# Narrower stationary operands in the capacity search, two more of its steps ahead of the expert stream, and a new table of spacings

## What is computed

```
def _moe2_ref(x, w_gate, w1, w2) -> np.ndarray:
    N, D = x.shape
    E = w_gate.shape[1]
    cap = N // E
    logits = x @ w_gate
    flat = logits.flatten()
    order = np.argsort(-flat)
    assigned = -np.ones(N, dtype=np.int64)
    counts = np.zeros(E, dtype=np.int64)
    for idx in order:
        tok, e = (int(idx) // E, int(idx) % E)
        if assigned[tok] >= 0 or counts[e] >= cap:
            continue
        assigned[tok] = e
        counts[e] += 1
        ...
    out = np.zeros((N, D), dtype=np.float32)
    for e in range(E):
        mask = assigned == e
        h = np.maximum(x[mask] @ w1[e], 0.0)
        out[mask] = h @ w2[e]
    return out.astype(np.float32)
```

## Time and profile before

| | us |
|---|---|
| median of 3 runs | 829.41 |
| lowest and highest | 829.33, 831.57 |
| profiled execution, its own time | 829.41 |
| its span, first to last instruction | 825.4 |
| PE busy | 727.5 |
| DVE busy | 359.0 |

### The profile page before, as it was taken

How to read it: one execution, slowest core, us unless ns; L and a number is a source line. 1 busy time by engine, 2 the same in 40 slices (tenths; PEclk the granted TensorE clock), 3 DMA queues, 4 the chain that set the end, 5 groups by cost and what they waited for, 6 DMA issues and landing times.

```text
span 825.4 us, 13873 instructions
## 1 busy us (share of the span) xinstructions
PE 727.5 (88%) x4561; PEld 504.0 (61%) x4561; DVE 359.0 (43%) x1458; ACT 220.7 (27%) x685; POOL 192.3 (23%) x251
## 2 busy tenths in 40 slices
PE   3788998998299999997219999999999999999995
PEld 2788988998287678675115555455555545555552
DVE  3577786886411121122583726537273563600000
ACT  2677787884011111111001111110211111021210
POOL 8275645452111111111010020202102020211001
PEclk9799999999599999999557999999999999999998
DMA  9898987587691618800033521507043160642000
GB/s 212 188 207 201 224 205 173 134 213 238 223 382 35 232 32 322 315 8 3 6 126 119 191 90 50 220 13 255 25 166 109 33 243 14 254 174 105 30 0 38
DMA packets 130466, 119.88 MB, mean 145 GB/s; under 512 B 95858, under 2 KB 95858, under 8 KB 130224
## 3 DMA queue, kind: packets, MB, share of 16 engines
q1 hardware_dynamic: 118192, 88.45, 35.2%
q10 hardware_dynamic: 6464, 14.73, 5.9%
q0 software_dynamic: 5760, 16.03, 5.7%
HBM read 105.95 MB, written 16.50 MB: 148 GB/s over the span
## 4 chain that ended last, share of the span: by engine, by line
PE 78%; DVE 9%; issue 3%; SPq 3%; DMA 3%; POOL 1%; ACT 1%; ACTq 0%; POOLq 0%; DVEq 0%
PE bank L1121 21%; PE bank L1136 21%; PE bank L1017 9%; PE bank L1034 8%; PE bank L877 3%; PE bank L898 3%; PE bank L1062 2%; PE bank L920 2%; SPq L465 2%; PE bank L887 2%; PE bank L1094 1%; DVE scratch L1346 1%; DVE shared L1357 1%; PE bank L997 1%; PE bank L864 1%
## 5 line engine op out<-in xcount | busy, mean ns | idle before, releaser
L1121 PE MATMUL bank<-scratch,weights 128*128 128x384 f32 x512 | 177.4, 499 | 0.7 <-ACT scratch L1302 0.7
L1136 PE MATMUL bank<-weights,scratch 128*128 128x512 f32 x384 | 175.2, 600 | 0.0
L1121 PEld LDWEIGHTS bank<-scratch,weights 128*128 128x128 f32 x512 | 94.3, 192 | 64.3 <-issue 9.8
L1136 PEld LDWEIGHTS bank<-weights,scratch 128*128 128x128 f32 x384 | 69.6, 190 | 70.7 <-issue 68.4
L1205 ACT ACTIVATE scratch<-shared,neg_max 128x120 f32<-128x120 f32 x192 | 73.4, 383 | 33.0 <-DVE neg_max L1357 20.9
L1308 ACT ACTIVATE scratch<-bank 128x384 f32<-128x384 f32 x64 | 31.4, 491 | 152.8 <-PE bank L1121 152.8
L664 POOL TENSOR_TENSOR scratch<-scratch,row_inv 128x480 f32<-128x480 f32 x48 | 47.3, 986 | 78.7 <-DVE row_inv L1367 78.5
L1017 PEld LDWEIGHTS bank<-mix,weights 128*128 128x128 f32 x512 | 60.8, 197 | 5.2 <-issue 5.2
L1017 PE MATMUL bank<-mix,weights 128*128 128x128 f32 x512 | 61.7, 279 | 1.5 <-DVE mix L1571 1.5
L822 POOL DMA_INDIRECT out<-scratch,idx x24 | 25.2, 1049 | 147.4 <-ACT scratch L1314 145.6
L1034 PE MATMUL bank<-weights,mix 128*128 128x512 f32 x128 | 58.2, 597 | 0.0
(11 more groups left out here) (225 smaller groups left out, 941.6 us busy)
## 6 DMA issues: line engine op xcount, KB each, us to landing
weights<-in_moe_w SPq DMA_DIRECT2D x20, 2048.0 KB, 8.3
scratch<-in_moe_w SPq DMA_DIRECT2D x8, 2048.0 KB, 15.5
weights<-in_moe_w ACTq DMA_DIRECT2D x16, 512.0 KB, 6.1
mix<-in_v SPq DMA_DIRECT2D x40, 192.0 KB
rows<-row SPq DMA_DIRECT2D x24, 264.5 KB, 3.6
weights<-in_k SPq DMA_DIRECT2D x24, 256.0 KB, 5.2
scratch<-in_q SPq DMA_DIRECT2D x24, 256.0 KB, 4.4
weights<-in_v ACTq DMA_DIRECT2D x24, 192.0 KB, 4.1
```

What stands on the lines that cost most here:

```text
L1121: last = mm(hb2[f % 2][:, 0:CAP], w1_sb[odd][:, c, f * P:(f + 1) * P], xT2[odd][:, c, :], start=(c == 0), stop=(c == C - 1), skip_group_ch ...
L1136: last = mm(yb2[c % 2][:, :], hT2[odd][:, f, c * P:(c + 1) * P], w2_sb[odd][:, f, :], start=(f == 0), stop=(f == FC - 1), skip_group_check ...
```

## The change

Four edits, all in the second mixture.

```
@@ -349,7 +349,7 @@
-        reach = row_hot
+        reach = row_hot[:, :, 0:KEYS, :]
@@ -1059,7 +1059,7 @@
-                        last = mm(counts[:, 0:E], reach[:, j // 2, :, j % 2], cand_h[:, j, :],
+                        last = mm(counts[0:ROUND_KEYS[r], 0:E], reach[:, j // 2, 0:ROUND_KEYS[r], j % 2], cand_h[:, j, :],
                                   start=(j == 0), stop=(j == NT - 1), skip_group_check=True)
@@ -1095,10 +1095,10 @@
-            AHEAD = 4
+            AHEAD = 6
             UP, DOWN = 3, 4
             TURN_AT = CT * FC - 6
-            spacing = [20, 9, 10, 6] + [14, 6] * (ROUNDS - 2) + [12, 12, 13, 17]
+            spacing = [18, 7, 8, 7] + [12, 8] * (ROUNDS - 2) + [15, 11, 8, 17]
@@ -1592,7 +1592,6 @@
             v_.memset(room_e, float(CAP))
-            v_.memset(reach, 0.0)
             link(v_.memset(assigned, 0.0))
@@ -1680,12 +1679,11 @@
                         plink(ins)
+                        v_.tensor_copy(digits_h[:, 0, :], digits_i[:, 0, :])
+                        plink(v_.tensor_scalar(digits_h[:, 1:, :], digits_i[:, 1:, :], 1.0, None, ALU.add))
                     dve.wait_ge(s.counted, 2 * ROUNDS * ph + 2 * r + 1)
                     v_.tensor_tensor(out=enough_h[0:wide_r, :], in0=counts[0:wide_r, 0:E], in1=room_e[0:wide_r, :],
                                      op=ALU.is_ge).then_inc(s.judged, 1)
-                    if r == 0:
-                        v_.tensor_copy(digits_h[:, 0, :], digits_i[:, 0, :])
-                        plink(v_.tensor_scalar(digits_h[:, 1:, :], digits_i[:, 1:, :], 1.0, None, ALU.add))
```

## The result

The changed kernel takes 864.84 us (median of 4 runs, 862.97 to 865.60) against 830.28 us for the kernel before in the same comparison. The ratio is 1.041, with a 95% interval of 1.039 to 1.043: 34.6 us slower, where 26.0 us had been forecast, and above the range, which ended at 862.

A forecast was written before the change was run, and what follows sets the result against it. TensorE's instructions bound the stream, and TensorE and VectorE taking turns bound the prelude. Terms 4.2 + 0.5 + 4.5 - 0.6 + 10.2 + 7.2 = +26.0 us on 829.41 gave 855.4 us, range 838 to 862.

The forecast's parts named there:

- Edit 1: Narrower count loads cost more on TensorE: +10.2 us in the stream, +4.2 us in the prelude before the added round.
- the fast load is lost: Count matmuls: bf16 loads of fewer than 128 columns lose the fast path; slow load with clock as it is, chance 0.62.
- Edit 2: No zeroing: the 1.34 us VectorE memset is covered by the transfer of the scores, so 0.
- Edit 3: Conversions earlier, ahead of round 0's judgement: about +0.25 us in phases 0 and 1, +0.5 us together; stream 0.
- Edit 4: AHEAD = 6: a whole round ahead of expert 0's transposes adds 4.5 us; its count and vote leave the stream, -0.6 us.
- Worth 1 us either way: Low-clock stretch of the first products: a shift in where the clock rises changes the time by 1 us.
- Edit 5: New spacings stall the stream 0.35 and 0.65 us before steps 11 and 12 in six phases, plus 1.2: +7.2 us.
- The vote of round 0: In the stream, a down product (0.88 us) between count and vote hides the judgement's wait behind the conversions: 0.
- the load keeps its price: Rival: narrow count loads cost no more than 128-column ones, +10.5 us, 840 us; chance 0.17.
- The clock did not rise in the prelude: Judges the rival that slow prelude counts lift the clock from 0.50 to 1.00: -8, 847 us; chance 0.09.
- overlapping loads: Rival: narrow count loads run beside the matmul ahead; at 5 ns per matmul in the stream, 827 us; chance 0.02.

The follow-up runs named there:

- e2: Kernel before with only the narrower count operand and no zeroing: 852.74 us against 829.65, ratio 1.027.
- e1: Changed kernel with count matmuls back at 128 stationary columns and the zeroing back: 840.28 us against 829.65 for the kernel before.
- e7: Kernel before with counts of 32, 64, 128, 128 and 128 stationary columns, zeroing kept: 840.13 us against 836.13, ratio 1.005.
- e5: Kernel before with only the two conversions of round 0 moved ahead of the wait for the counts: 836.37 us against 836.13.
- e12: Second run of the kernel before with only the round-0 conversions moved earlier: 833.35 us against 833.22, ratio 1.001.
- e9: Kernel before, unchanged, run again on the second chip: 832.74 us against 833.22, ratio 1.000.
- e4: Kernel before with only AHEAD raised from 4 to 6, old spacings, full width: 830.66 us against 829.65, ratio 1.003.
- e3: Kernel before with only the new table of spacings, AHEAD = 4: 833.55 us against 829.65, ratio 1.006.
- e11: Kernel before with the new spacings and AHEAD = 6 together, full width, late conversions: 841.51 us against 833.22, ratio 1.010.
- e10: Changed kernel, no further edit, run again on the second chip: 865.63 us against 833.22 for the kernel before, ratio 1.038.
- e13: Kernel before with the vote of round 0 one down product later (spacing 13, not 9): 833.27 us against 836.25, ratio 0.996.

## Why the prediction was wrong

The direction was right, and so were the mechanisms in the sum, but the price of the narrow loads was too low and some costs were missing from it; the total was 8.6 us short of the measured 34.6, or 6.4 short of the 32.4 on one chip, and the range missed by 3 us. Term by term, from the traces of the changed kernel:

- **Edit 1, "half the f32 price: 50 ns at full clock, 100 ns at half clock, for 127 columns; half of that for 63 (25 and 50); no change for 31."** This step failed in its size. Measured: (1.56 - 0.20) / 23 = 59 ns and (2.72 - 0.24) / 23 = 108 ns for 127 columns, (0.96 - 0.17) / 23 = 34 ns and (1.44 - 0.19) / 23 = 54 ns for 63. At full clock a group of 24 gains 0.81 us, not 0.60, and 63 and 31 columns gain 0.30 and 0.09 us, not 0. In the stream that is 17 x 0.81 + 5 x 0.30 + 5 x 0.09 = 15.7 us for the 10.2 forecast, the largest part of the miss; in the prelude 3 x 1.38 + 2 x 0.5 = 5.1 for 4.2. The products beside the 31- and 63-column counts add the 1.1 us of e2, for 0 forecast. I had halved a price that was itself read off rows with 17 and 120 moving columns, and had put 56 ns no further out than the edge. At full clock the pace goes from 34 ns for 63 columns to 59 for 127, so 64 columns make 25 ns; 127 at that rate are 49 ns, close to the 50 forecast, and some 10 ns do not go by the width. At half clock it goes from 54 to 108 ns, with next to nothing over. What the 10 ns are, no run here shows.
- **That the fast load is lost** was right, and e1, e2 and e7 show it. By the rule of the Trainium skill (TensorE: Matmul & The Clock Gate, section Weight-path perf modes — Fast Weight Load (FWL) and DoubleRow) only 128 weights of a type other than FP32 load fast; the rows of 31, 32, 63, 64, 127 and 128 columns agree in that only 128 keeps the old price of a count. The gain that the section gives, about twofold, is 59 against 25 ns here at full clock; at half clock the trace has more, 108 against 26.
- **Edit 2, 0** and **Edit 3, +0.5.** The zeroing was covered, VectorE now waits 7.20 us for the scores in place of 5.32. The conversions cost 0.3 us in each of phases 0 and 1, as forecast (e1 has both without a late signal); the late signal adds 0.5 us in phase 1. In their times e5 and e12 can't be told from before.
- **Edit 4, +4.5 in the prelude, -0.6 in the stream.** The transposes come 5.10 us after the vote of round 1 (451.83 - 446.73) where it was 0.35 before, so +4.75 (against e9, whose transposes waited 0.53 us for their rows, +4.4). "Worth 1 us either way" for the clock was too narrow: e4 gained 2.6 us by it.
- **Edit 5, stalls of 0.35 and 0.65 us.** From step 10 to 11 the trace has 475.99 - 473.61 = 2.38 us where three products take 2.03, and from 11 to 12 it has 2.66: 0.35 and 0.63. In expert 5 the stall ahead of step 12 of phase 7 is 0.73 us of idle time, 0.8 us from start to start, and not 1.2; the six phases and this one lose 6.7 us for the 7.2 forecast. The place and size held; that the table works only together with AHEAD was in the positions, but unsaid, and e3 and e11 show it.
- **The vote of round 0** was not in the sum. "TensorE has a down product (0.88 us) between count and vote there: 0" fails with 0.5 us of idle time in five phases, 3.1 us from start to start. It is no cost of the change where before has it as well, but counts against the changed kernel where the comparison is with a run that has it not.

Together, from the first count to the end:

- The first pair of traces, prelude: 5.1 for the counts, 0.6 for the conversions, 0.5 for the late signal, 4.75 for the added round, and 0.5 between step 11 of phase 0 and the first count of phase 1, which e2 has too, which no term foresaw and whose cause is open. In all 11.45 us, measured 11.4.
- The first pair, stream: 15.7 - 0.6 + 1.1 for the counts and the products beside them, 6.7 for the stalls of edit 5, 3.1 for the late vote. In all 26.0 us, measured 26.0.
- On one chip (e9 to e10), stream: 15.7 - 0.6 + 1.1 + 6.7, then -0.7 for the vote and -0.4 for the clock, which rises 4.6 us behind the first product and not 5.4. In all 21.8 us, measured 21.8.

The first pair of traces gives 37.4 us for both stages, where its medians give 34.6; what makes up the difference is open.

Of the rivals, "the load keeps its price" gave 840 us for a kernel that e1 then made, at 840.28. The clock did not rise in the prelude: it stood at 0.50 until 460.6 us, 5.2 us behind the first product. Nothing pointed to overlapping loads.

## What to carry to other kernels

In counts like these (groups of 24 matmuls with 8 moving columns, at full clock) a bf16 stationary operand of 128 columns was cheaper than one of 31, 32, 63, 64 or 127: pad it and ignore the surplus outputs, unless the reader of the surplus costs more. When a unit of filler is a whole matmul, a spacing table means nothing by itself; work out at which product each step falls, for the same starting step, and set it against the helper engine's chain. Count a stall from start to start of the records, not by the idle time in the brackets. And a price for an operation that the trace does not have should be taken from a row that is like it in every part, or have its range widened by the part that differs.

## What the runs showed of the hardware

- A count matmul with 8 moving columns and a bf16 stationary operand takes, per matmul in a row of 24: at full clock 25 ns for 128 columns, about 26 for 31, 34 for 63, 59 for 127; at half clock 26 ns for 128, 54 for 63 and 108 for 127. The group of 31 takes 0.69 us to the next product and that of 128 takes 0.60, and a group of 31 or 63 makes the two records beside it 0.11 us longer.
- In all nine traces of the second chip (e5 to e13), and in the first one of the changed kernel, the signal of the round-0 counts of phases 2 to 6, which end while GpSimd issues indirect DMAs, comes 1.2 to 3.0 us after them; in e1 to e4 on the first chip, and in the first trace of before, it comes at once. The cause is open.
- The granted clock rose 0.6 us ahead of the first product (e4) or 3.5 to 5.9 us behind it (all others) in kernels that differ by a few us in the prelude, which is worth up to 2.6 us here.
